# Two-layer gated network on one core: new instruction sequences for the first two chunks and the drain

## What is computed

```python
w = softmax(weight * 1, axis=-1)                 # 8 heads x 7 taps
x = causal 7-tap convolution of x, per head      # 2 x 4096 tokens
x = (sigmoid(x @ w_gate) * (x @ w_val)) @ w_out  # 192 -> 1536 -> 192
h = x @ w_in                                     # 192 -> 2048
P = a0 + a1*h + a2*h**2 + a3*h**3
Q = 1 + |b0|*|h| + |b1|*h**2
out = (P / (Q + 1e-6)) @ w_out2                  # 2048 -> 192
```

## Time and profile before

| what | value |
|---|---|
| time, median of 3 executions | 1352.86 us (1352.71 to 1354.04) |
| profiled execution, its own time | 1354.07 us |
| its span, first to last instruction | 1352.2 us |
| mean granted TensorE clock | 0.987 of full |
| busy: PE, DVE, ACT, POOL | 1285.2, 1257.9, 1105.6, 658.5 us |
| first matmul | 15.84 us |

### The profile page before, as it was taken

How to read it: one execution, slowest core, us unless ns; L and a number is a source line. 1 busy time by engine, 2 the same in 40 slices (tenths; PEclk the granted TensorE clock), 3 DMA queues, 4 the chain that set the end, 5 groups by cost and what they waited for, 6 DMA issues and landing times.

```text
span 1352.2 us, 16870 instructions
## 1 busy us (share of the span) xinstructions
PE 1285.2 (95%) x5440; PEld 1027.0 (76%) x5440; DVE 1257.9 (93%) x1201; ACT 1105.6 (82%) x1278; POOL 658.5 (49%) x337
## 2 busy tenths in 40 slices
PE   4889999999999999999999999999999999999776
PEld 3767788787877878787787878778787887888654
DVE  7759999999999999999999999999999999998898
ACT  5468788888888789788888979888898888889674
POOL 1423545444555544564564555455455455554432
PEclk9899999999999999999999999999999999999898
DMA  7100000010000001000000000001000000000000
GB/s 207 35 0 20 1 8 25 1 32 0 12 20 8 24 0 31 0 12 20 8 24 0 17 14 12 20 0 31 0 12 20 8 23 0 20 0 12 1 12 12
DMA packets 15960, 23.66 MB, mean 18 GB/s; under 512 B 2240, under 2 KB 10048, under 8 KB 15936
## 3 DMA queue, kind: packets, MB, share of 16 engines
q1 hardware_dynamic: 14160, 21.30, 5.7%
q10 hardware_dynamic: 1776, 2.06, 0.6%
HBM read 13.13 MB, written 6.29 MB: 14 GB/s over the span
## 4 chain that ended last, share of the span: by engine, by line
PE 83%; DVE 10%; issue 4%; ACT 2%; DMA 0%; DVEq 0%; POOL 0%; ACTq 0%; SPq 0%
PE up_ps L303 10%; PE up_ps L305 10%; PE up_ps L304 10%; PE up_ps L307 9%; PE up_ps L306 9%; PE acc_main L310 7%; PE acc_main L313 7%; PE acc_main L311 7%; PE acc_tail L312 7%; PE acc_tail L314 7%; DVE numer L1152 1%; DVE tail_twice L1109 1%; DVE frac_high L1170 1%; DVE numer L1160 1%; DVE denom L1189 1%
## 5 line engine op out<-in xcount | busy, mean ns | idle before, releaser
L971 POOL TENSOR_TENSOR frac_low<-denom,seed 128x1024 fp32r<-128x1024 f32 x126 | 374.6, 2973 | 567.8 <-DVE denom L1189 558.5
L962 POOL TENSOR_TENSOR gated_low<-gated,gated_high 128x512 fp32r<-128x512 f32 x192 | 265.7, 1402 | 109.0 <-ACT gated_high L657 108.9
L303 PE MATMUL up_ps<-x_high,up_high 128*128 128x512 f32 x640 | 259.1, 405 | 54.3 <-DVE denom L1142 19.3
L305 PE MATMUL up_ps<-x_low,up_high 128*128 128x512 f32 x640 | 253.7, 396 | 0.0
L304 PE MATMUL up_ps<-x_high,up_low 128*128 128x512 f32 x640 | 253.7, 396 | 0.0
L307 PE MATMUL up_ps<-x_tail_low,up_tail 128*128 128x512 f32 x640 | 252.7, 395 | 0.0
L306 PE MATMUL up_ps<-x_tail_high,up_tail 128*128 128x512 f32 x640 | 252.6, 395 | 0.0
L303 PEld LDWEIGHTS up_ps<-x_high,up_high 128*128 128x128 f32 x640 | 122.0, 191 | 97.0 <-DVE denom L1142 26.3
L677 ACT ACTIVATE numer<-up_ps,coef 128x1024 f32<-128x1024 f32 x128 | 153.9, 1202 | 40.2 <-PE up_ps L307 38.0
L1152 DVE TENSOR_TENSOR numer<-up_ps,numer 128x1024 f32<-128x1024 f32 x128 | 156.4, 1222 | 29.6 <-ACT seed L668 20.6
L686 ACT ACTIVATE up_ps<-up_ps 128x1024 f32<-128x1024 f32 x128 | 129.4, 1011 | 54.4 <-DVE numer L1160 52.3
(11 more groups left out here) (86 smaller groups left out, 2279.9 us busy)
## 6 DMA issues: line engine op xcount, KB each, us to landing
x_raw<-x_chunks SPq DMA_DIRECT2D x16, 393.0 KB, 3.1
out_chunks<-out_main SPq DMA_DIRECT2D x16, 256.0 KB, 2.1
tail_twice<-conv SPq DMA_DIRECT2D x60, 64.0 KB, 2.0
out_chunks<-tail_part SPq DMA_DIRECT2D x16, 128.0 KB, 2.3
numer<-w_out SPq DMA_DIRECT2D x1, 1536.0 KB, 7.1
seed<-w_out ACTq DMA_DIRECT2D x1, 1152.0 KB, 12.5
denom<-w_in SPq DMA_DIRECT2D x2, 512.0 KB, 4.9
denom<-w_gate SPq DMA_DIRECT2D x1, 576.0 KB, 5.5
```

The source lines that it names most:

```text
L303: nc.tensor.matmul(acc, up_high[:, cols], x["high"][:], start=True, stop=False)
L305: nc.tensor.matmul(acc, up_high[:, cols], x["low"][:], start=False, stop=False)
L962: nc.gpsimd.tensor_tensor(gated_low[:, b], gated[:, b], gated_high[:, b], ALU.subtract).then_inc(gated_low_done, 1)
L971: nc.gpsimd.tensor_tensor(ring(frac_low, j, 2, LOW_RING), ring(denom, j), ring(seed, j), ALU.mult).then_inc(frac_low_done, 1)
```

## The change

The lists of PE, ACT, POOL and DVE for chunks 0 and 1 and for the drain are written in another order. `chunk(i)`, every function, every wait's condition and SP's list stay, and each list still has the same calls. The core of the diff (PE; the change of chunk and the first pairs on DVE; POOL; the drain on ACT and DVE):

```diff
--- before.py
+++ after.py
@@ -399,55 +399,55 @@
             up_gate(0, 1, 2)
             up_val(0, 1, 0)
             up_val(0, 1, 1)
+            down_gated(0, 0, 0)
             up_val(0, 1, 2)
-            down_gated(0, 0, 0)
             down_gated(0, 0, 1)
+            up_gate(0, 2, 0)
             down_gated(0, 0, 2)
-            up_gate(0, 2, 0)
             up_gate(0, 2, 1)
             up_gate(0, 2, 2)
+            down_gated(0, 1, 0)
+            down_gated(0, 1, 1)
             up_val(0, 2, 0)
             up_val(0, 2, 1)
             up_val(0, 2, 2)
-            down_gated(0, 1, 0)
-            down_gated(0, 1, 1)
-            down_gated(0, 1, 2)
             up_gate(0, 3, 0)
             up_gate(0, 3, 1)
+            down_gated(0, 1, 2)
             up_gate(0, 3, 2)
             up_val(0, 3, 0)
+            down_gated(0, 2, 0)
             up_val(0, 3, 1)
             up_val(0, 3, 2)
-            down_gated(0, 2, 0)
             down_gated(0, 2, 1)
             down_gated(0, 2, 2)
+            down_gated(0, 3, 0)
+            down_gated(0, 3, 1)
             up_gate(1, 0, 0)
             up_gate(1, 0, 1)
+            down_gated(0, 3, 2)
             up_gate(1, 0, 2)
             up_val(1, 0, 0)
-            down_gated(0, 3, 0)
-            down_gated(0, 3, 1)
-            down_gated(0, 3, 2)
             up_val(1, 0, 1)
             up_val(1, 0, 2)
             up_h(1, 1, 0)
...
@@ -713,91 +713,91 @@
...
             round_gated(0, 3, 0)
             round_x0_tail(1)
-            round_weights_main("out2", 0)
-            round_weights_tail("out2", 0)
+            sigmoid(0, 3, 2)
             round_gated(0, 3, 1)
+            round_x0_main(1)
             round_gated(0, 3, 2)
+            copy_x1_part(1)
             sigmoid(1, 0, 0)
-            copy_x1_part(1)
             sigmoid(1, 0, 1)
             round_x1_main(1)
             sigmoid(1, 0, 2)
             round_x1_tail(1)
             round_gated(1, 0, 0)
...
@@ -882,63 +882,63 @@
 
 
             sigmoid(chunks - 1, 3, 2)
+            round_gated(chunks - 1, 3, 0)
             log_table()
+            log(*late(-3))
             exp(*late(-4))
-            round_gated(chunks - 1, 3, 0)
-            log(*late(-3))
+            round_gated(chunks - 1, 3, 1)
             slope(*late(-2))
+            round_gated(chunks - 1, 3, 2)
             magnitude(*late(-2))
             exp(*late(-3))
-            round_gated(chunks - 1, 3, 1)
+            magnitude(*late(-1))
             slope(*late(-1))
-            round_gated(chunks - 1, 3, 2)
             square(*late(-2))
-            magnitude(*late(-1))
             log(*late(-2))
+            square(*late(-1))
+            copy_x1_part(chunks)
             exp(*late(-2))
-            copy_x1_part(chunks)
             round_x1_main(chunks)
-            square(*late(-1))
             round_x1_tail(chunks)
             log(*late(-1))
+            exp(*late(-1))
             magnitude(*late(0))
             slope(*late(0))
-            exp(*late(-1))
+            slope(*late(1))
             square(*late(0))
-            slope(*late(1))
             magnitude(*late(1))
...
@@ -980,9 +980,9 @@
             split_gated(0, 2, 0)
             split_gated(0, 2, 1)
             split_gated(0, 2, 2)
-            split_x0_main(1)
             split_gated(0, 3, 0)
             split_gated(0, 3, 1)
+            split_x0_main(1)
             split_gated(0, 3, 2)
             split_gated(1, 0, 0)
             split_gated(1, 0, 1)
@@ -1023,8 +1023,8 @@
 
             split_gated(chunks - 1, 2, 2)
             low_fraction(*late(-6))
+            split_gated(chunks - 1, 3, 0)
             low_fraction(*late(-5))
-            split_gated(chunks - 1, 3, 0)
             split_gated(chunks - 1, 3, 1)
             split_gated(chunks - 1, 3, 2)
             low_fraction(*late(-4))
...
@@ -1224,94 +1224,94 @@
             split_weights("val", 0)
             split_weights("gate", 1)
 
+            split_weights_main("val", 1)
             gate(0, 0, 0)
+            split_weights_tail("val", 1)
             gate(0, 0, 1)
             gate(0, 0, 2)
-            split_weights_main("val", 1)
-            split_weights_tail("val", 1)
             split_weights_main("out1", 0)
             split_weights_tail("out1", 0)
             conv_tap(1, 0)
+            gate(0, 1, 0)
+            gate(0, 1, 1)
             conv_tap(1, 1)
             conv_tap(1, 2)
             conv_tap(1, 3)
-            gate(0, 1, 0)
-            gate(0, 1, 1)
+            split_weights_main("in", 0)
             gate(0, 1, 2)
+            gate(0, 2, 0)
             conv_tap(1, 4)
-            gate(0, 2, 0)
             gate(0, 2, 1)
             gate(0, 2, 2)
-            split_weights_main("in", 0)
-            split_weights_tail("in", 0)
-            split_weights_main("in", 1)
-            split_weights_tail("in", 1)
             conv_tap(1, 5)
             conv_tap(1, 6)
+            split_weights_tail("in", 0)
             gate(0, 3, 0)
+            split_weights_main("in", 1)
             gate(0, 3, 1)
+            split_weights_tail("in", 1)
+            split_x0_tail(1)
             gate(0, 3, 2)
-            split_x0_tail(1)
+            conv_tap(2, 0)
             split_weights_main("out2", 0)
             split_weights_tail("out2", 0)
             sum_x1_tail(1)
+            gate(1, 0, 0)
+            split_x1_main(1)
             split_x1_tail(1)
-            split_x1_main(1)
-            gate(1, 0, 0)
+            conv_tap(2, 1)
             gate(1, 0, 1)
             gate(1, 0, 2)
-            conv_tap(2, 0)
-            conv_tap(2, 1)
+            conv_tap(2, 2)
             quadratic(1, 1, 0)
             cubic(1, 1, 0)
-            conv_tap(2, 2)
             quadratic(1, 1, 1)
+            cubic(1, 1, 1)
             denominator(1, 1, 0)
-            cubic(1, 1, 1)
+            conv_tap(2, 3)
             denominator(1, 1, 1)
-            conv_tap(2, 3)
...
@@ -1390,47 +1390,47 @@
             chunk_loop(dve, chunk)
 
 
+            denominator(*late(-2))
             product(*late(-4))
-            denominator(*late(-2))
+            cubic(*late(-1))
             rest(*late(-4))
-            cubic(*late(-1))
+            denominator(*late(-1))
             sum_x1_tail(chunks)
             split_x1_main(chunks)
             split_x1_tail(chunks)
-            denominator(*late(-1))
+            high_fraction(*late(-2))
             product(*late(-3))
-            high_fraction(*late(-2))
+            product(*late(-2))
             rest(*late(-3))
-            product(*late(-2))
+            high_fraction(*late(-1))
             quadratic(*late(0))
```

149 lines of the change are left out of this document (74 added, 75 removed).

## The result

| | before | after |
|---|---|---|
| time, median | 1352.78 us (4 runs, 1352.09 to 1354.04) | 1335.84 us (4 runs, 1334.76 to 1336.79) |
| ratio | | 0.9873 (95%: 0.9856 to 0.9891) |
| profiled execution, its span | 1354.07, 1352.2 us | 1335.3, 1333.5 us |
| mean granted clock | 0.987 | 0.991 |
| busy: PE, DVE, ACT, POOL | 1285.2, 1257.9, 1105.6, 658.5 us | 1279.1, 1252.3, 1104.9, 658.5 us |

The kernel is 16.9 us faster; 1336.0 was forecast.

The account below looks back on a forecast made before the run. PE was taken to bound the repeated chunk, DVE the drain. Of 23.7 us ahead of the loop, 15.4 net plus 1.5 in the drain gave 16.9 off 1354.07, 1337.2; adjusted to the median, 1336.0 (54%), range 1332 to 1343.

Parts of the forecast that it names:

- (a): Chunk 0, before up_val(0,1,0): the wait for DVE's split of w_val goes, gain 1.14 us.
- (b): Before up_gate(1,0,0): the 3.60 us wait for chunk 1's x0 goes, with 2.98 of clock, gain 6.58 us.
- (c): Before up_h#1: the wait for the end of the x1 chain goes, gain 1.52 us.
- (d): Before up_gate(1,1,0): the wait for denominator #1 grows from 3.53 to 5.0 us; loss 2.2 with clock.
- (e): Before up_gate(1,2,0): more cover for denominator #3's 2.63 us wait; gain 1.6 us and 1.7 of clock.
- (f): Before up_gate(2,0,0): the 3.13 us wait for denominator #7 goes, with 1.70 of clock, gain 4.83 us.
- (g): Before the loop on PE: five waits fewer spare about 0.16 us each, 0.8 us.
- (h): Chunk 2: 0.6 us given back for waits like those of each later period.
- (i): Drain: DVE's 2.17 us wait goes, exp #117 delayed about 0.6; gain 1.5 us, bounds 0 to 3.3.
- contention: Rival: denser DVE work meets POOL's three times more, at 1.4 us each; cost 4.2, 1340 us, 15%.
- third rival: x0 or x1 comes late all the same, a wait with half clock returns: 6.6 us on top, 1342.6 us, 15%.
- slower ring: At x0: late POOL split_x0_main(1) holds up PE's up_gate(1,0,0) and DVE's list at once; 1356 us, 3%.

Follow-up runs that it names:

- drain only: Kernel before with only the drain's lists new, chunks 0 and 1 keeping their old lists: 1351.62 us, ratio 0.9985.
- DVE's old list: Changed kernel with DVE's old list for chunk 0, up to conv_tap(2, 1), put back: 1346.06 us, ratio 0.9944.
- POOL's old place: Changed kernel with POOL's split_x0_main(1) back ahead of split_gated(0,3,0) and (0,3,1): 1343.26 us, ratio 0.9923.
- chunk 1 only: Kernel before with new lists only for chunk 1 from the first hidden pair on, old drain: 1347.96 us, ratio 0.9959.
- quarter splits: Changed kernel with POOL's split_gated writing 128 of 512 columns, the rest zero: 1332.9 us, one execution.
- the shorter chain: Changed kernel with one down ahead of up_gate(1,1,0), denominator #1 before cubic #2, log #1 before square #2, drain's exp #117 first: 1335.68 us, ratio 0.9869.

## Why the prediction was right, and where it was not

The frame held: a fixed period of 79.80 us, a head to win from, a drain bound by DVE. The 23.7 us to win were those of one execution; 8.1 of them were clock, which the same lists did not pay in full in drain only. Point by point:

- (a) right. No wait before up_val(0,1,0); with DVE's old list it is back with 1.13 us.
- (b) right, and as close as said. 57.6 was walked for x0 and for PE; they were 58.63 and 58.70, both later by the 0.5 us by which PE started later and by 0.5 more. The run with POOL's old place shows what this meeting was worth: 6.6 to 7.4 us, of the size of the 6.58 of this step. Its 2.98 of clock are one execution's: behind the same wait 13 matmuls ran slow there and 8 in drain only and in chunk 1 only.
- (c) right. x1 ready at 66.71, PE at 66.82 (walked: 65.6, 65.7). (a) to (c) were 9.24 together and measured 9.34, or 9.86 without the later start.
- (d) right in the wait: 5.0 walked, 4.91 measured. The clock's part was no fixed number: one execution of this list showed 2.95 us of work at half clock, another 4.57, so 1.48 or 2.3 us; 2.4 was taken, by a row of the drain.
- (e) The wait for denominator #3 is gone, as is the stretch at half clock. The pieces were one wait of 0.67 us, by POOL, where 1.0 was taken. (d) and (e) together gained 2.12 us (up_h#5 starts 39.80 us behind up_h#1 before, 37.68 after) for 1.1 walked; of the 1.0 more, 0.9 is that smaller loss of clock in (d).
- (f) right: 4.83 walked, 4.98 measured. Behind up_h#1 the gain was 2.11 us at up_gate(1,3,0) (51.34 to 49.23), 5.46 at up_gate(2,0,0) (75.41 to 69.95) and 7.09 at up_gate(3,0,0) (155.62 to 148.53): 3.35 up to the wait and 1.63 behind it. All of the 1.63 was taken for the half clock that had stood there. In drain only, with the old lists and full clock at that place, chunk 2 took 79.25 us against 80.21 before and 78.58 after, so the clock is 0.96 of it and the rest something else. The margin was 0.8 us as said. A lead from chunk 0 is not the cause: with chunk 1's lists alone the wait is gone too. What fits is the part of (f) on fractions #1 to #3: high_fraction #1 (86.07) and product #1 (88.47) now stand ahead of quadratic #3 (90.98), and DVE's wait there fell from 3.75 to 1.01 us. No run moved these alone. DVE's idle time from 19 us to denominator #7 fell from 30.9 to 19.7 us.
- (g) The 0.8 is inside the milestones and can't be read apart. (h) failed: nothing was given back in chunk 2; the lead of 14.80 us at up_gate(2,0,0) was 16.43 at up_gate(3,0,0), and stayed there.
- (i) mis-sized: 1.5 walked, 2.3 in the profiles, 2.05 by medians, inside its bounds of 0 to 3.3. DVE's idle time in the last 90 us fell from 5.15 to 2.60 us: the 2.17 before quadratic #120 are 0.07, and 0.44 before the sums of x1 are gone. The 0.6 us given to exp #117 cost nothing.

In the sum the forecast was 1.0 us short in the head (0.9 of clock in (d), 0.6 in (h), less the later start of 0.5) and 0.5 to 0.8 short in the drain. Between the two profiled executions, which the walk describes, the gain is 18.8 us and not 16.9. That the medians differ by 16.9 as well, and that 1336.0 meets 1335.84, is in part luck: the two errors were made up for by an execution of before that lay 1.3 us above its median and one of after 0.5 below.

Of the rivals, contention went the other way: DVE's busy time fell by 5.6 us with the same instructions. The part that the denser packing should have added did not come. The run with quarter splits puts 4.4 us in 1252 on three quarters of the gated splits' work; low_fraction, which POOL runs for 377 us and beside which the loop's lengthened operations lie, was left as it was, so the price of contention as a whole stays open. The changeover (third rival) stayed away with nothing to spare, and the two runs in which it came cost 6.6 and 9.4 us (7.4 and 10.2 against 1335.84) where the rival said 6.6. The slower ring did not occur, but a kernel slower than before does lie in this change: it is PE's list without the others, by 6.2 us: 1.5 through downs that were put ahead as cover and were not ready, the rest where cover was given up in chunk 1 while the late results stayed late.

## What to carry to other kernels

Work moved ahead of a wait as cover must itself be ready by then: look at who makes its inputs and at what stands before them on that engine's list, and move all lists together, since one of them alone may cost as much as the whole brings. A wait that survives its cover being moved about, with nearly the same sum in other places, points to the chain behind it. For many executions of one period, compare starts of the same instruction in two traces: pieces of 0.1 to 0.2 us that no view of waits lists can add up to more than a visible wait.

## What had not been expected

The same list with the same wait of 4.91 us drew 3.4 us at half clock in one execution and 6.8 us in another, 0.8 us of difference in the lead; another 0.65 came from the first matmuls of the kernel, which ran slow for 7 in the one and 13 in the other. And the length of a wait alone did not tell whether the clock fell: beside 2.63 us before up_gate(1,2,0) it fell in the kernel before and stayed at full in drain only, whose lists are the same there; beside 2.63 us before up_gate(1,1,0) with the shorter chain it stayed at full, and fell beside the 1.82 us that came 17 us later. What decides between them is open.
